# Second products of an expert's first layer issued two blocks behind the first products, and other blocks for some of the first expert's weight splits

## The reference

```
logits = x @ w_gate                      # 3072 x 8
# tokens in descending order of logit go to an expert until it holds 384
for e in range(8):
    h = relu(x[mask_e] @ w1[e])          # 384 -> 1024
    out[mask_e] = h @ w2[e]              # 1024 -> 384
h = relu(x @ w_in)                       # 384 -> 2048
return h * h @ w_out                     # 2048 -> 384
```

## Time and profile before

| | |
|---|---|
| median of 3 runs | 811.03 us (810.62 to 811.88) |
| the profiled execution's own time | 812.36 us |
| its span, first to last instruction | 810.6 us |
| PE busy | 777.7 us, 96% of the span |
| DVE, ACT, POOL busy | 500.7, 321.5, 292.9 us |
| mean granted clock of PE | 0.978 |

### The profile page before, as it was taken

How to read it: one execution, slowest core, us unless ns; L and a number is a source line. 1 busy time by engine, 2 the same in 40 slices (tenths; PEclk the granted TensorE clock), 3 DMA queues, 4 the chain that set the end, 5 groups by cost and what they waited for, 6 DMA issues and landing times.

```text
span 810.6 us, 19168 instructions
## 1 busy us (share of the span) xinstructions
PE 777.7 (96%) x6971; PEld 743.8 (92%) x6971; DVE 500.7 (62%) x1195; ACT 321.5 (40%) x718; POOL 292.9 (36%) x295
## 2 busy tenths in 40 slices
PE   8999994799999999999999999999999999999996
PEld 6999993589899999999999999999999999999995
DVE  7988886788846783678367837783777336721210
ACT  4556654313532353235323532363236324531332
POOL 7766640102631163116311631263126312621333
PEclk9999996699999999999999999999999999999998
DMA  8878744502300140013001300130013002300000
GB/s 227 263 233 239 236 126 177 183 3 79 108 1 30 40 145 0 29 49 136 0 29 51 133 0 29 55 129 0 29 56 128 0 30 79 108 1 30 0 1 30
DMA packets 22196, 65.27 MB, mean 81 GB/s; under 512 B 3664, under 2 KB 6736, under 8 KB 22160
## 3 DMA queue, kind: packets, MB, share of 16 engines
q1 hardware_dynamic: 19088, 55.34, 21.4%
q0 software_dynamic: 3072, 9.44, 3.3%
HBM read 55.33 MB, written 9.44 MB: 80 GB/s over the span
## 4 chain that ended last, share of the span: by engine, by line
PE 79%; DVE 10%; issue 4%; POOL 3%; ACT 1%; DMA 1%; POOLq 0%; SPq 0%; DVEq 0%; ACTq 0%
PE bank L1362 14%; PE bank L1366 14%; PE bank L1363 14%; PE bank L1420 7%; PE bank L1421 7%; PE bank L1422 7%; PE bank L1166 3%; PE bank L1204 3%; PE bank L1179 3%; DVE hot L863 2%; DVE hot L977 1%; PE bank L1233 1%; PE bank L1220 1%; PE bank L1241 1%; POOL xg L476 1%
## 5 line engine op out<-in xcount | busy, mean ns | idle before, releaser
L503 POOL TENSOR_TENSOR h_lo<-sq,h_hi 128x384 fp32r<-128x384 f32 x128 | 155.4, 1217 | 377.3 <-DVE sq L1076 377.2
L1076 DVE SCALAR_TENSOR_TENSOR sq<-bank,relu 128x384 f32<-128x384 f32 x128 | 71.0, 555 | 152.1 <-ACT relu L627 150.1
L627 ACT ACTIVATE relu<-bank 128x384 f32<-128x384 f32 x128 | 62.9, 492 | 196.1 <-PE bank L1366 182.5
L1420 PE MATMUL bank<-m_hi,h_hi 128*128 128x384 f32 x384 | 132.7, 346 | 2.2 <-POOL h_lo L503 2.0
L1362 PE MATMUL bank<-x_hi,m_hi 128*128 128x384 f32 x384 | 129.8, 338 | 0.6
L1421 PE MATMUL bank<-m_lo,h_hi 128*128 128x384 f32 x384 | 130.2, 339 | 0.0
L1366 PE MATMUL bank<-x_hi,m_lo 128*128 128x384 f32 x384 | 130.0, 339 | 0.0
L1422 PE MATMUL bank<-m_hi,h_lo 128*128 128x384 f32 x384 | 129.8, 338 | 0.0
L1363 PE MATMUL bank<-x_lo,m_hi 128*128 128x384 f32 x384 | 128.9, 336 | 0.0
L621 ACT ACTIVATE h_hi<-bank 128x384 fp32r<-128x384 f32 x64 | 31.5, 492 | 175.3 <-PE bank L1366 175.3
L1068 DVE SCALAR_TENSOR_TENSOR h_lo<-bank,h_hi 128x384 fp32r<-128x384 f32 x64 | 35.4, 554 | 73.2 <-ACT h_hi L621 73.2
(11 more groups left out here) (191 smaller groups left out, 1445.3 us busy)
## 6 DMA issues: line engine op xcount, KB each, us to landing
w_raw<-we_in SPq DMA_DIRECT2D x48, 512.0 KB, 5.5
nn<-nn_in SPq DMA_DIRECT2D x24, 384.0 KB, 4.0
tt<-tt_in SPq DMA_DIRECT2D x44, 192.0 KB, 4.3
m_raw<-m_in SPq DMA_DIRECT2D x12, 512.0 KB, 6.1
x_rows<-yrow SPq DMA_DIRECT2D x24, 192.0 KB, 2.2
tt<-tt_in SPq DMA_DIRECT2D x4, 256.0 KB, 5.9
xg<-x_rows,perm_next POOLq DMA_INDIRECT x24, 5.1
out<-xg,perm_now POOLq DMA_INDIRECT x24, 2.6
```

What stands on the lines that cost most here:

```text
L503: pool.tensor_tensor(h_lo[g % 3][:, :], sq[g % 2][:, :], h_hi[g % 3][:, :].bitcast(f32), ALU.subtract).then_inc(lo2_ready, 1)
L627: act.activation(relu[:, :], h_ps[g % 3][:, 0:CAP], ACT.Relu).then_inc(relu_ready, 1)
L1076: dve.scalar_tensor_tensor(out=sq[g % 2][:, :], in0=h_ps[g % 3][:, 0:CAP], scalar=0.0, in1=relu[:, :], op0=ALU.max, op1=ALU.mult).then_inc ...
L1420: pe.matmul(acc_ps[t][:, 0:DM], h_hi[r][:, s], m2_hi[:, c:c + DM], start=first, stop=False)
```

## The change

Three things move. On PE, step g of the first layer issues `contract(g - 2)` in place of `contract(g - 1)`, and step 7 issues `contract(5)`, `contract(6)` and `contract(7)` one after the other; this holds for all eight experts. The counts and `add_full` stay in their steps. For the first expert alone, ACT and DVE split weight tile 3 after block 0's relu and its low part instead of before it, and DVE splits tile 4 in step 2 (before: ahead of step 1) and tile 5 in step 4 (before: step 3). And the twelve halves of `out_low` go from steps 2, 3, 4, 5, 8, 10, 13, 15, 16, 17, 18 and 19 to steps 8 (three), 10 (three), 17, 18 and 19 (two each). The number of instructions of each kind stays as it is.

```diff
-OUT_LOW_AT = [2, 3, 4, 5, 8, 10, 13, 15, 16, 17, 18, 19]
+OUT_LOW_AT = [8, 8, 8, 10, 10, 10, 17, 17, 18, 18, 19, 19]
...
             for d in range(DC):
                 x_high(0, d)
-            split_high(0, W1_TILES)
...
             high(0, 0)
-            for j in range(W1_TILES + 1, WE_TILES):
+            for j in range(W1_TILES, WE_TILES):
                 split_high(0, j)
...
             for d in range(DC):
                 x_low(0, d)
-            split_low(dve, 0, W1_TILES)
...
-                        if is_first(i) and g == 3:
-                            split_low(dve, 0, W1_TILES + 2)
-                        if is_first(i) and g in OUT_LOW_AT:
-                            out_low(dve, OUT_LOW_AT.index(g)).then_inc(out_lo_ready, 1)
+                        if is_first(i) and g in (2, 4):
+                            split_low(dve, 0, W1_TILES + g // 2)
+                        if is_first(i):
+                            for n in range(2 * OUT_TILES):
+                                if OUT_LOW_AT[n] == g:
+                                    out_low(dve, n).then_inc(out_lo_ready, 1)
...
             low(0, 0)
-            split_low(dve, 0, W1_TILES + 1)
+            split_low(dve, 0, W1_TILES)
...
-                    if g < G1:
+                    if 1 < g < G1:
+                        contract(i, g - 2)
+                    if g == G1 - 1:
                         contract(i, g - 1)
-                    if g == G1 - 1:
                         contract(i, g)
                     if g > G1 + 1:
                         contract(i, g - 2)
```

## The result

The changed kernel takes 823.54 us (median of 4, 822.82 to 825.04), the kernel before 811.45 beside it: ratio 1.0143, 95% interval 1.0126 to 1.0161. That is 12.1 us slower; 10.2 were forecast, and 821.2 us. The median lies at the upper edge of the range given, 823.5; put on the median of 811.03 from which the forecast started, the loss of 12.1 makes 823.1. The profiled execution of it took 825.04 us with a span of 823.3.

What follows compares the result with a forecast made beforehand. Later experts were taken as bound by PE's own work, so the change could only add waits. Terms 6.2 + 1.6 + 0.0 + 1.7 + 0.7 = 10.2 us on 811.03 gave 821.2 us, range 816.5 to 823.5.

Steps and rivals of the forecast that it cites:

- PE's order in experts two to six: At count(0, 0), PE arrives a block earlier and waits for DVE's unmoved comparison: 1.25 us per expert, 6.2 in five.
- nothing takes it back later: From hidden(3) through step 7 of experts two to six, no later wait shrinks, so the 1.25 us loss per expert stays.
- The first expert's first layer: One block lost at the count, +1.6 us, and a clock fall behind its wait of about 3 us, +1.7.
- the swap of splits and halves: First expert's first layer, steps 2 to 6: moved DVE work cancels out, worth 0.0 us, with 0.3 either way.
- The first expert's second layer: Block 15's saving of 3.6 us against new waits of 3.5 and half a clock fall: +0.7, bounds -1.8 and +1.6.
- The wait at block 15: First expert's second layer: 1.95 us wait for POOL's h_lo goes with its slow stretch as halves leave steps 13, 15, 16: -3.6.
- the sum: First expert's second layer: three halves in steps 8 and 10 make PE wait 1.5 us at ranks, 2.0 more at slot_ids.
- the clock's fall: First expert's second layer: the 2.0 us wait at slot_ids may lower the clock; half of 1.66 us was added.
- Rival 1: Faster, 805.8 us: compare(0, 0) ends by two blocks after hidden(1), the deciding point, so first-expert waits go; chance 0.05.
- Rival 2: No change, 811 us: a later wait in each expert takes in the lost block; chance 0.05.
- Rival 3: The clock falls at the count in every search expert: 8.3 us more, 829.5; chance 0.1.
- Rival 4: First expert kinder, no clock fall and no POOL in between: 6.0 us loss, 817.0; within the forecast's 0.8.

Runs made afterwards that it cites:

- after_again: The changed kernel run once more with no edit, for a second profile: 822.45 us, ratio 1.0136.
- filled: The changed kernel with 32 unread matmuls on PE in the first expert's wait, between contract(0) and count(0, 0), that expert taken out of PE's loop: 820.27 us, ratio 1.012.
- pe_only: The kernel before with only PE's new order; splits and halves stay where they were: 819.12 us, ratio 1.0078.
- dve_only: The changed kernel with PE's old order; the moved splits and halves stay: 815.80 us, ratio 1.0041.
- low_behind: The changed kernel with DVE's low part of block 1 issued behind compare(0, 0) in the six search experts: 813.85 us, ratio 1.0031.

## Why the prediction was right, point by point

**PE's order in experts two to six: right in its mechanism, a little too large in size.** Forecast 5 x 1.25 = 6.2 us; measured 5.3 (5.2 in after_again). The wait at the count is as worked out: from `hidden(1)` to `hidden(3)` the second expert takes 260.57 - 254.30 = 6.27 us, against 253.53 - 246.93 = 6.60 before, so `hidden(3)` is 0.33 earlier with a block less done. What failed is the sentence that nothing takes it back later. In step 7 the kernel before had lost 0.2 us at `count(1, 2)`, from the last `contract` to `hidden(8)`: 273.36 - 271.28 = 2.08 us. With three `contract` in a row ahead of it, it is 281.78 - 279.89 = 1.89. Five times 0.2 is the 1.0 us by which the forecast was too high. pe_only and dve_only show that this term belongs to PE's order alone, and low_behind that it is the distance to the end of the comparison.

**The first expert's first layer: forecast +3.3 (1.6 for the block, 1.7 for the clock), measured +3.8 and +3.6.** The comparison did stay where it was and the block was lost. The clock cost more than one fall was priced at: filled gives 2.2 to 2.4 us. The price was read from one fall of eleven slow matmuls, in a slow stretch of under 4 us; here it lasted about 7. Without the fall, in filled, the layer is 1.4 us longer than before, so the swap of splits and halves was worth about 0 as forecast, but not in the way forecast: PE's wait for `add_full` in step 6 grew from 0.19 to 0.69 us, and that in step 5, 0.73 us, went.

**The first expert's second layer: forecast +0.7, measured +1.6.** The wait at block 15 went with its slow stretch, -3.6 as forecast, but not by the halves alone, as the end of this point shows. DVE's three halves took what was worked out, 0.8 us of POOL among them (timelines of DVE and POOL):

```profile
198.13 2.71 DVE L288 TENSOR_TENSOR m_lo<-m_raw,m_hi 128x512 fp32r<-128x512 f32 x3
```

```profile
198.40 1.30 POOL L503 TENSOR_TENSOR h_lo<-sq,h_hi 128x384 fp32r<-128x384 f32 x1 [39.50 <-DVE sq L1074]
```

Three alone would take 3 x 0.6 + 0.08 = 1.9. This is the exclusive lock on the shared port pair of the Trainium skill's page "SBUF — State Buffer", section "SBUF: two separate sides"; the rows agree, with POOL's subtract lying inside DVE's 2.71 us.

At `ranks` the sum was right: it starts 204.53 - 194.98 = 9.55 us behind `hidden(8)`, against 197.36 - 189.22 = 8.14 before, 1.4 later where 1.5 stood. At `slot_ids` it was too large: `contract(12)` behind it is 216.22 - 194.98 = 21.24 us behind `hidden(8)`, against 207.54 - 189.22 = 18.32, 2.9 later where 3.5 stood. Two thirds of its matmuls ran ahead of the wait of 1.24 us, and the sum had put all of them behind.

Two things were too small. The halves of step 17 made PE wait 0.67 us, which stood only in the range. And the clock's fall was taken at half of 1.66 us. Five profiles have these steps of the halves. In three (the changed kernel twice, and filled) the clock fell behind the wait at `slot_ids`, to 0.50 in the slowest stretch; in dve_only and low_behind the same wait, 1.24 and 1.25 us, left it at 1.00. The second layer takes 59.3 us in the three and 58.1 and 58.2 in the two, so a fall costs 1.2 net. It costs less than its slow stretch because of block 15. Where the clock stayed, PE still waits 1.02 us there for POOL's `h_lo`; where it fell, PE comes later and that wait is gone. So at the full clock the moved halves shorten the wait at block 15 from 1.95 to 1.02 us, and the whole -3.6 came only together with the fall. Taking half was fair as a chance; the term was still 0.9 too small.

**The rest.** The sum of the three stages is 10.7 us in the first profile and 10.4 in the second, against 10.2 forecast. That this is so close is partly luck: the later experts came out 0.9 to 1.0 lower than forecast, the first expert's two layers 1.2 to 1.4 higher. The medians differ by 12.1 and 10.9. In the profile of the kernel before, the block 15 fall had cost 1.6 us, and pe_only shows that an execution can go without it; 810.28 and 818.0 are both executions of that one kernel. What of the 12.1 is such chance can't be settled from two profiles; the 2.0 us ahead of the experts in the first profile were chance.

**The rivals.** Rival 1 did not happen, but its one point of decision was the right one: low_behind moves the comparison and brings most of the time back, 4.6 of 5.3 us in the later experts. Rival 2 has its 0.2 us in each expert and no more. Rival 3, a fall of the clock at every count, did not happen: between 240 and 600 us the clock is 1.00 in the changed kernel, with two waits of 0.37 and 0.56 us in each expert. No run here shows the falling clock in every pass that the Trainium skill's page "TensorE: Matmul & The Clock Gate" describes in its section "HAM oscillation — how this bites in real kernels"; it was paid only at the first expert's longer waits. Rival 4 did not happen either.

## What to carry to other kernels

When work is issued further behind on the busy engine, look at what else stands in its order, here a small product that belongs to another chain: with a block less ahead of it, the margin of 0.2 us became two waits of 0.9 us together in each of five experts, and three of 3.2 in the first. The cure was on the other engine, where the new order had made one operation less urgent; it could go behind the one that had become urgent. And count several operations in a row at more than their sum where another engine gets in between: three halves took 2.71 us where three alone would take 1.9, and what DVE had to do behind them came late. Last, test each part of a change alone: here the steps of the halves held nearly all there was to gain.

## What the runs showed of the hardware that was not expected

The same wait of 1.95 us at block 15 made the clock fall to 0.50 in the profile of before and left it at 1.00 in that of pe_only. A wait of 1.24 us behind small matmuls, with PE busy for 2.76 of 4 us, made it fall in the changed kernel, and again in after_again and filled; the same wait in dve_only, with PE busy for 2.79 of 4 us, left it alone:

```profile
212.00:216.00 4.00, 2.76 (x30) 2.51 (x28) 4.00 (x5) 2.41 (x5) 2.29 (x2) 1.00 0.00 0
...
218.00:220.00 2.00, 2.00 (x8) 2.00 (x7) 1.93 (x7) 0.00 (x0) 1.18 (x1) 0.50 0.44 131
```

```profile
209.90:213.90 4.00, 2.79 (x30) 2.54 (x28) 4.00 (x5) 2.40 (x5) 2.29 (x2) 1.00 0.00 0
214.00:216.00 2.00, 2.00 (x19) 2.00 (x20) 2.00 (x2) 0.86 (x1) 0.75 (x1) 1.00 0.00 0
```

The first two lines are the changed kernel's, the last two those of dve_only. So neither the length of one wait nor PE's busy time around it tells whether the clock falls, and what decides is not shown. One profile gives the price of a fall only to within a factor: 1.5 to 2.4 us here.
